# The second MLP of a three-layer kernel on one core: hidden units first and whole, then a down projection by seven block products

## The chip, the cores and the metric

One core of a Trainium2 chip. The metric is the device time of one execution in microseconds (us). TensorE is PE in the profile (its weight loads are PEld), VectorE is DVE, ScalarE is ACT, GpSimd is POOL, SyncE is SP.

## What is computed

Retention attention on q, k, v (2 batches, 8 heads, 768 positions, 64 per head) gives x of 2 x 768 x 512. Then a mixing layer and an MLP, cut to what matters:

```python
theta = x @ w_theta
y = einsum('ts,bsd->btd', w_tok_r, x * cos(theta)) + einsum('ts,bsd->btd', w_tok_i, x * sin(theta))
u = x + y
x = u + maximum(u @ w_ch, 0)                      # the channel layer
h = maximum(x.T @ w_tok1, 0) @ w_tok2             # per batch, over the 768 tokens, inner width 256
u = x + h.T
out = u + maximum(u @ w_ch1, 0) @ w_ch2           # the second MLP: 512 -> 1536 -> 512
```

## The kernel before

All activations stay on chip, channels on the partitions (NK = 4 blocks of 128), tokens along the free axis. Float32 operands are split in two parts, high (ACT, a rounding copy) and low (DVE or POOL, value less high), and each product is three matmuls of the parts: high by high, high by low, low by high (`three`, L780). Every engine's program is written out by hand in order, with semaphores between the engines.

In order of time: twelve attention chunks (g = 0 to 11) with theta, sine and cosine; the token mixing (`mix`), which is done with seven block products (STEPS = 28, 72 matmuls of 384 columns a product); the channel layer (`channels(q)`, q = 0 to 15), with turns of its result onto the other axis (`turn_x2`) from q = 9 on; `tokens_up`, `tokens_down`; and the second MLP.

In the attention start, ACT's first instruction of use is `x_high(0)` (L477), then two `theta_high` (L460); DVE does `x_low(0)` (L618) and two `theta_low` (L578), on which `theta(0)` of TensorE waits. `weigh(g)` (L594) multiplies the scores of a chunk by the decay.

`channels(0)` waits for y_kept of all 28 mixing steps, which DVE's `keep_y` (L687 at the end) signals.

The second MLP goes over three tiles of 512 tokens: batch 0's first 512, batch 1's first 512, and the last 256 of both. In each tile there are NF = 12 blocks of inner units. `hidden(tile, f)` makes one (12 matmuls of 512 columns into a PSUM bank), ACT takes its relu as high part (L561), DVE the low part (L768), and `down(tile, f)` adds its share to four banks of sums (12 matmuls of 512 columns), one block behind. After the 12th block DVE adds the four sums to res (L774) and SP sends them (L365).

Weights come in 17 pieces of 1024 columns through three stage buffers. ACT and DVE split the first five during the mixing, POOL splits the others (L373, L375): those of w_ch2 and w_ch1, in `w_a`, `ch2_a` and `w_b`. POOL also does the low parts `ut_low` (L400) ahead of the channel layer and `u2_low` (L406) ahead of the second MLP. In the mixing, POOL's queue makes sums of weight quarters by DMAs that add to what lies in `raw` (L420 to L437).

## Time and profile before

| | |
|---|---|
| median of 3 runs | 449.81 us (449.34 to 450.46) |
| profiled execution | 449.38 us, span 447.6 us |
| PE busy | 437.8 us, 98% of the span, 2676 matmuls |
| PEld busy | 382.3 us |
| DVE busy | 210.4 us |
| ACT busy | 127.9 us |
| POOL busy | 99.1 us |

The span is from the first to the last instruction of the profiled execution; its time holds 1.8 us more, which lies outside. Busy time of an engine is the union of its instructions. Consecutive matmuls overlap in the records (each lasts longer than the distance to the next), so the distance between starts is the price of one in a stream.

### The profile page before, as it was taken

To read this page: it belongs to the slowest core of one execution; us is meant where nothing else is said; L and a number is where in the kernel's file an instruction comes from. 1 tells how busy PE (TensorE), PEld (TensorE's weight loads), DVE (VectorE), ACT (ScalarE), POOL (GpSimd) and SP (SyncE) were. 2 spreads that over 40 slices of the span, in tenths; PEclk is the share of its full clock that TensorE was granted. 3 is DMA by queue.
4 is the path that set the end of the run, shared out by engine and by line. 5 is a ranking of instruction groups with operands and counts; after the bars stand their busy time and mean duration, and the time that the engine had idled before them with its cause. 6 is when DMAs were issued, how large, how long until landed. Compare 5 with 4: busy or idle time off the path is not lost.

```text
span 447.6 us, 6232 instructions
## 1 busy us (share of the span) xinstructions
PE 437.8 (98%) x2676; PEld 382.3 (85%) x2676; DVE 210.4 (47%) x304; ACT 127.9 (29%) x194; POOL 99.1 (22%) x80
## 2 busy tenths in 40 slices
PE   7799999999999999999999999999999999999996
PEld 4587878899999999999889888888888888888885
DVE  3789998799999993244335211112211113111113
ACT  0455654734455456012313211111111110111110
POOL 2422241000200009940998940000000000000000
PEclk9999999999999999999999999999999999999999
DMA  8955697540784111030241000000200001000002
GB/s 309 395 218 202 267 235 168 105 142 0 183 182 154 47 49 48 13 129 1 94 142 47 1 0 1 0 0 12 84 1 0 0 1 73 21 1 0 1 0 94
DMA packets 9980, 38.29 MB, mean 86 GB/s; under 512 B 993, under 2 KB 2145, under 8 KB 8161
## 3 DMA queue, kind: packets, MB, share of 16 engines
q1 hardware_dynamic: 7856, 28.31, 17.3%
q0 software_dynamic: 1952, 9.44, 9.2%
q8 instruction: 21, 0.34, 0.3%
q10 hardware_dynamic: 144, 0.14, 0.1%
q14 instruction: 7, 0.05, 0.0%
HBM read 34.75 MB, written 3.15 MB: 85 GB/s over the span
## 4 chain that ended last, share of the span: by engine, by line
PE 95%; DVE 2%; DMA 1%; ACT 1%; issue 0%; DVEq 0%; ACTq 0%
PE ps L780 85%; PE ps L797 3%; PE ps L837 3%; PE ps L851 2%; PE ps L927 1%; PE ps L811 1%; PE ps L827 1%; DMA qkv_in<-qkv 1%; DVE w_sq L578 1%; DVE res L774 1%; DVE prob L594 1%; ACT L477 0%; ACT w_sq L460 0%; ACT x_hi L477 0%; DVE res L613 0%
## 5 line engine op out<-in xcount | busy, mean ns | idle before, releaser
L780 PE MATMUL ps<-u,w_a 128*128 128x512 f32 x432 | 103.3, 389 | 0.0
L768 DVE SCALAR_TENSOR_TENSOR w_sq<-ps,w_sq 128x512 fp32r<-128x512 f32 x36 | 24.9, 692 | 156.7 <-ACT w_sq L561 156.7
L780 PEld LDWEIGHTS ps<-u,w_a 128*128 128x128 f32 x432 | 81.1, 188 | 16.8
L780 PE MATMUL ps<-tw,zs 128*128 128x384 f32 x504 | 88.1, 334 | 0.0
L780 PEld LDWEIGHTS ps<-tw,zs 128*128 128x128 f32 x504 | 87.3, 188 | 0.1
L561 ACT ACTIVATE w_sq<-ps 128x512 fp32r<-128x512 f32 x36 | 21.6, 599 | 168.0 <-PE ps L780 168.0
L780 PE MATMUL ps<-w_sq,ch_a 128*128 128x512 f32 x216 | 51.9, 389 | 0.0
L780 PE MATMUL ps<-w_sq,w_b 128*128 128x512 f32 x216 | 51.4, 389 | 0.0
L780 PEld LDWEIGHTS ps<-w_sq,w_b 128*128 128x128 f32 x216 | 40.5, 188 | 8.4
L780 PEld LDWEIGHTS ps<-w_sq,ch_a 128*128 128x128 f32 x216 | 40.5, 188 | 8.4
L780 PE MATMUL ps<-ut,w_sq 128*128 128x384 f32 x192 | 35.6, 339 | 0.7 <-issue 0.7
L504 ACT ACTIVATE zs<-z 128x768 fp32r<-128x768 f32 x28 | 23.7, 846 | 37.0 <-PE ps L780 37.0
L780 PEld LDWEIGHTS ps<-ut,w_sq 128*128 128x128 f32 x192 | 32.9, 188 | 1.0 <-issue 1.0
L780 PE MATMUL ps<-w_sq,x_hi 128*128 128x512 f32 x96 | 30.8, 402 | 2.3 <-DVE w_sq L578 2.3
L400 POOL TENSOR_TENSOR ut<-res,ut 128x384 fp32r<-128x384 f32 x16 | 16.6, 1068 | 33.0 <-ACT ut L509 33.0
L780 PEld LDWEIGHTS ps<-w_sq,x_hi 128*128 128x128 f32 x96 | 17.1, 188 | 5.9 <-issue 2.2
L584 DVE TENSOR_TENSOR tw<-raw,tw 128x768 fp32r<-128x768 f32 x21 | 20.8, 988 | 0.0
L780 PE MATMUL ps<-w_sq,x_lo 128*128 128x512 f32 x48 | 18.8, 392 | 0.0
L385 POOL TENSOR_TENSOR k_dec<-qkv_in,cst 128x512 f32<-128x512 f32 x10 | 11.5, 1148 | 30.7 <-DMA qkv_in<-qkv 26.8
L731 DVE SCALAR_TENSOR_TENSOR res<-ps,res 128x384 f32<-128x384 f32 x16 | 8.9, 558 | 19.3 <-PE ps L780 19.3
L467 ACT ACTIVATE tw<-raw 128x768 fp32r<-128x768 f32 x21 | 17.4, 830 | 1.0 <-DMA raw<-tok 1.0
L780 PE MATMUL ps<-u,w_b 128*128 128x512 f32 x72 | 17.4, 395 | 0.0
(83 smaller groups left out, 473.1 us busy)
## 6 DMA issues: line engine op xcount, KB each, us to landing
qkv_in<-qkv SPq DMA_DIRECT2D x11, 1024.0 KB, 6.1
stage<-weights SPq DMA_DIRECT2D x17, 512.0 KB, 3.3
raw<-tok POOLq DMA_DIRECT2D x7, 1152.0 KB, 8.9
cols_out<-res SPq DMA_DIRECT2D x12, 256.0 KB, 2.1
raw<-tok SPq DMA_DIRECT2D x6, 384.0 KB, 8.1
raw<-tok POOLq DMA_DIRECT2D x3, 384.0 KB, 9.2
qkv_in<-qkv SPq DMA_DIRECT2D x2, 512.0 KB, 5.0
raw<-theta_w SPq DMA_DIRECT2D x2, 512.0 KB, 8.6
```

The source lines that it names most:

```text
L385: pool.tensor_tensor(heads(k_dec[:, n % 2, :]), heads(qkv_in[:, g % NQ, 2 * DM:3 * DM]), key_decay, ALU.mult).then_inc(key_ready, 1)
L400: pool.tensor_tensor(u_half(1, b, k, half), res_half(b, k, half), f32(u_half(0, b, k, half)), ALU.subtract).then_inc(ut_lo, 1)
L467: act.activation(tw[:, p % 2, 0, at], raw[:, W_RAW[p], at], ACT.Copy).then_inc(tok_hi, 1)
L504: act.activation(zs[:, s % NZ, 0, :], z[:, Z_KIND[p], i, :], ACT.Copy, scale=Z_SIGN[p]).then_inc(z_hi, 1)
L561: act.activation(h2[:, f % 2, 0, :], bank(BK_H2 + f % 4), ACT.Relu).then_inc(h2_hi, 1)
L584: dve.tensor_tensor(tw[:, p % 2, 1, at], raw[:, W_RAW[p], at], f32(tw[:, p % 2, 0, at]), ALU.subtract).then_inc(tok_lo, 1)
L731: dve.scalar_tensor_tensor(out=part, in0=ps[:, BK_M + q % 2, 0:HS], scalar=0.0, in1=part, op0=ALU.max, op1=ALU.add).then_inc(x2_kept, 1)
L768: dve.scalar_tensor_tensor(out=h2[:, f % 2, 1, :], in0=bank(BK_H2 + f % 4), scalar=0.0, in1=f32(h2[:, f % 2, 0, :]), op0=ALU.max, op1=ALU. ...
L780: mm = pe.matmul(dst, left(l), right(r), start=first and n == 0, stop=last and n == 2, skip_group_check=True)
L797: mm = pe.matmul(ps[:, BK_SCORE + r, i * P:(i + 1) * P], qkv_in[rows, g % NQ, DM + i * P:DM + (i + 1) * P], qkv_in[rows, g % NQ, i * P:(i ...
L837: mm = pe.matmul(ps[cols, BK_Y + r, i // 2 * P:(i // 2 + 1) * P], qkv_in[:, g % NQ, 3 * DM + h * D:3 * DM + (h + 1) * D], prob[:, r, i * P ...
L851: mm = pe.transpose(ps[:, BK_XROW, k * P:(k + 1) * P], res[:, b, k, c * P:(c + 1) * P], ident)
```

## The change

Three edits.

1. ACT runs a sine over one column of the zeroed tile `idle` at its very start, before it waits for the constants.
2. The wait for y_kept of all 28 steps moves from `channels(0)` to `turn_x2(0)`.
3. The second MLP is in two parts. First all 36 `hidden` blocks (12 matmuls of 512 columns each, in the order of HIDDEN, eight PSUM banks in turn). ACT (`first_units`) keeps relu of batch 0, DVE (`second_units`) that of batch 1 less another block, unsplit, in `h_a` and `h_b`. Then seven products p, each of four cells i (an output block of 128 channels and 384 tokens), each cell of 6 x 3 = 18 matmuls of 384 columns. The inner axis is halved, the output channels are halved, and the batches are the third pair. Each product needs one operand of sums of hidden units (`h_sums`, DVE), split by `h_op_high` (ACT) and `h_op_low` (DVE) in six parts of 768 columns, and one operand of sums of w_ch2 quarters of 1536 columns, split by `w2_high` and `w2_low`. The sums of weights are made by POOL's adding DMAs in `w2_raw`. A cell's result is added by DVE (`keep_down`) to one or three places of res. Operands of product p + 1 are made while product p runs; each operand has two buffers. w_ch1 is no longer held whole: its six pieces go through the three places of `ch1`, the last three split by POOL when the places come free. There are 11 pieces; w_ch2 is loaded apart from them, 768 KB a quarter.

The constants are NPHI = NF // 2 = 6 and W2C = 2 * NPHI * P = 1536; MIDDLE, the first piece that POOL splits, is now P_CH1. `hidden_units(f_half, phi, b)` is a slice of `h_a` (phi below 4) or `h_b`; `h_op(p, phi)` one of 12 places in `h_ops_a`, `h_ops_b`, `h_ops_c`, the last of which lies over `u`. `parts_of(b, n)` counts the units of batch b kept by the first n blocks; `hidden_kept(eng, n)` waits for block n to have been taken from its bank.

```diff
+DOWN = 7
+CELLS = 4
+H_PLACE = ((0, 0), (1, 0), (1, 1), (0, 0), (1, 0), (0, 1), (0, 0))
+H_SUMS = (3, 4, 6)
+W2_RAW = (0, 1, 0, 1, 1, 1, 0)
+W2_SIGN = (1.0, 1.0, 1.0, -1.0, -1.0, 1.0, -1.0)
+HIDDEN = [(f, 0) for f in range(4)] + [(f, t) for f in range(4) for t in (1, 2)] + [
+    (f, t) for f in range(4, NF) for t in range(TILES)]
...
-BK_SUM, BK_H2 = 0, 4
+BK_H2 = (1, 2, 4, 5, 3, 6, 7, 0)
+BK_DOWN = (0, 0, 4, 4, 4, 0, 0)
...
             sp.wait_ge(zi_ready, NG)
             for i in range(N_PIECES):
                 load_piece(i)
-            for tile in range(TILES):
-                for n in range(NK):
-                    sp.wait_ge(sum_kept, tile * NK + n + 1)
-                    to = out[tile, n, :, 0:DM] if tile < B else out[:, n, :, DM:S].rearrange("b p t -> p b t")
-                    sp.dma_start(to, tokens(tile, n)).then_inc(out_sent, 16)
-            sp.wait_ge(out_sent, 16 * TILES * NK)
+            split_done(sp, N_PIECES - 1)
+            for i in range(2):
+                sp.dma_start(w2_raw[:, i, :], ch2[i]).then_inc(w2_in[i], 16)
+            for p, r, b in ((1, 0, 0), (4, 1, 0), (5, 1, 1), (6, 0, 1)):
+                for i in range(CELLS):
+                    m, half = i // 2, i % 2
+                    sp.wait_ge(down_kept, p * CELLS + i + 1)
+                    sp.dma_start(out[b, 2 * r + m, :, half * HS:(half + 1) * HS],
+                                 res_half(b, 2 * r + m, half)).then_inc(out_sent, 16)
+            sp.wait_ge(out_sent, 16 * 4 * CELLS)
...
                     for k in range(NK):
                         ut_low(b, k, half)
             pool.wait_ge(mix_ready, STEPS)
-            for i in range(P_CH2A, P_CH1):
...
+            for i in range(P_CH1, P_CH1 + NSTAGE):
                 split_piece(i)
             u2_low(0)
             u2_low(1)
...
+                f = 2 * (i - P_CH1 - NSTAGE) + 1
+                pool.wait_ge(h2_ready, HIDDEN.index((f, 2)) + 1)
                 split_piece(i)
+            def load_w2(i, q, sent):
+                pool.dma_start(w2_raw[:, i, :], ch2[q]).then_inc(sent, 16)
+            def add_w2(i, q, sent):
+                pool.dma_start(w2_raw[:, i, :], ch2[q], accum_op=ALU.add).then_inc(sent, 16)
+            pool.wait_ge(w2_lo, 1)
+            add_w2(0, 2, s2_part)
+            pool.wait_ge(s2_part, 16)
+            add_w2(0, 3, s2_w_in)
+            pool.wait_ge(w2_lo, 2)
+            load_w2(1, 0, w2_11_again)
+            pool.wait_ge(w2_11_again, 16)
+            add_w2(1, 2, s3_w_in)
+            pool.wait_ge(w2_lo, 3)
+            add_w2(0, 1, s4_w_in)
+            pool.wait_ge(w2_lo, 4)
+            load_w2(1, 3, w2_22_in)
+            pool.wait_ge(w2_lo, 5)
+            add_w2(1, 2, s1_w_in)
...
+            act.wait_ge(idle_ready, 1)
+            act.activation(spare[:, :], idle[:, 0:1], ACT.Sin)
             act.wait_ge(const_in, 16)
             for g in range(NG + 2):
...
-            def h2_high(tile, f):
-                act.wait_ge(h2_ready, tile * NF + f + 1)
-                act.activation(h2[:, f % 2, 0, :], bank(BK_H2 + f % 4), ACT.Relu).then_inc(h2_hi, 1)
+            def first_units(n):
+                f, tile = HIDDEN[n]
+                cols = slice(0, DM) if tile == 0 else slice(DM, S)
+                act.wait_ge(h2_ready, n + 1)
+                act.activation(hidden_units(f % 2, f // 2, 0)[:, cols], bank(BK_H2[n % 8])[:, 0:cols.stop - cols.start],
+                               ACT.Relu).then_inc(h2_first, 1)
+            def h_op_high(p, phi):
+                half, b = H_PLACE[p]
+                if p in H_SUMS:
+                    act.wait_ge(h_sum, H_SUMS.index(p) * NPHI + phi + 1)
+                elif b:
+                    act.wait_ge(h2_second, parts_of(1, HIDDEN.index((2 * phi + half, 2)) + 1))
+                else:
+                    act.wait_ge(h2_first, parts_of(0, HIDDEN.index((2 * phi + half, 2)) + 1))
+                if p == 1 or p == 0 and phi >= 4:
+                    act.wait_ge(h2_ready, len(HIDDEN))
+                elif p >= 2:
+                    act.wait_ge(down_ready, (p - 1) * CELLS)
+                act.activation(h_op(p, phi)[:, 0, :], hidden_units(half, phi, b), ACT.Copy).then_inc(h_op_hi, 1)
+            def w2_high(p):
+                act.wait_ge((w2_in[0], w2_in[1], s2_w_in, s3_w_in, w2_22_in, s1_w_in, s4_w_in)[p], 16)
+                if p == 0:
+                    act.wait_ge(h2_ready, HIDDEN.index((9, 2)) + 1)
+                elif p == 1:
+                    act.wait_ge(h2_ready, len(HIDDEN))
+                else:
+                    act.wait_ge(down_ready, (p - 1) * CELLS)
+                act.activation(w2[:, p % 2, 0, :], w2_raw[:, W2_RAW[p], :], ACT.Copy,
+                               scale=W2_SIGN[p]).then_inc(w2_hi, 1)
...
-            for tile in range(TILES):
-                for f in range(NF):
-                    h2_high(tile, f)
+            for n in range(len(HIDDEN)):
+                f, tile = HIDDEN[n]
+                if tile != 1:
+                    first_units(n)
+                if tile == 2 and f % 2 and f < 8:
+                    h_op_high(0, f // 2)
+                if (f, tile) == (10, 2):
+                    w2_high(0)
+            h_op_high(0, 4)
+            h_op_high(0, 5)
+            for p in range(1, DOWN):
+                w2_high(p)
+                for phi in range(NPHI):
+                    h_op_high(p, phi)
...
-                    dve.tensor_tensor(part, as_tokens(tile, bank(BK_SUM + n)), part, ALU.add).then_inc(sum_kept, 1)
+            def second_units(n):
+                f, tile = HIDDEN[n]
+                half, phi = f % 2, f // 2
+                cols, at = (slice(0, DM), 0) if tile == 1 else (slice(DM, S), S - DM)
+                less = hidden_units(0, phi, half)[:, cols]
+                dve.wait_ge(h2_ready, n + 1)
+                if tile == 2:
+                    dve.wait_ge(h2_first, parts_of(0, n + 1))
+                elif half == 0:
+                    dve.wait_ge(h2_first, parts_of(0, HIDDEN.index((f, 0)) + 1))
+                else:
+                    dve.wait_ge(h2_second, parts_of(1, HIDDEN.index((f - 1, 1)) + 1))
+                if tile == 2 and half:
+                    dve.wait_ge(h2_second, parts_of(1, HIDDEN.index((f - 1, 2)) + 1))
+                dve.scalar_tensor_tensor(out=hidden_units(half, phi, 1)[:, cols],
+                                         in0=bank(BK_H2[n % 8])[:, at:at + cols.stop - cols.start], scalar=0.0,
+                                         in1=less, op0=ALU.max, op1=ALU.subtract).then_inc(h2_second, 1)
+            def h_op_low(p, phi):
+                half, b = H_PLACE[p]
+                dve.wait_ge(h_op_hi, p * NPHI + phi + 1)
+                dve.tensor_tensor(h_op(p, phi)[:, 1, :], hidden_units(half, phi, b), f32(h_op(p, phi)[:, 0, :]),
+                                  ALU.subtract).then_inc(h_op_lo, 1)
+            def h_sums(p, phi):
+                t1, t2 = hidden_units(0, phi, 1), hidden_units(1, phi, 1)
+                to = hidden_units(*H_PLACE[p][:1], phi, 0)
+                dve.wait_ge(h_op_lo, (0, 0, 0, 0, 1, 0, 3)[p] * NPHI + phi + 1)
+                if p == 6:
+                    dve.tensor_tensor(to, t2, t1, ALU.add).then_inc(h_sum, 1)
+                else:
+                    dve.wait_ge(h2_second, parts_of(1, HIDDEN.index((2 * phi + 1, 2)) + 1))
+                    dve.tensor_tensor(to, t2, to, ALU.subtract).then_inc(h_sum, 1)
+            def w2_low(p):
+                dve.wait_ge(w2_hi, p + 1)
+                what, hi, lo = w2_raw[:, W2_RAW[p], :], w2[:, p % 2, 0, :], w2[:, p % 2, 1, :]
+                if W2_SIGN[p] > 0:
+                    dve.tensor_tensor(lo, what, f32(hi), ALU.subtract).then_inc(w2_lo, 1)
+                else:
+                    dve.scalar_tensor_tensor(out=lo, in0=what, scalar=-1.0, in1=f32(hi), op0=ALU.mult,
+                                             op1=ALU.subtract).then_inc(w2_lo, 1)
+            def keep_down(p, i):
+                m, half = i // 2, i % 2
+                r11, r12 = (res_half(b, m, half) for b in range(B))
+                r21, r22 = (res_half(b, 2 + m, half) for b in range(B))
+                got = ps[:, BK_DOWN[p] + i, 0:HS]
+                dve.wait_ge(down_ready, p * CELLS + i + 1)
+                if p == 0:
+                    dve.tensor_tensor(r12, r12, got, ALU.add)
+                    dve.tensor_tensor(r21, r21, got, ALU.subtract)
+                    dve.tensor_tensor(r22, r22, got, ALU.subtract).then_inc(down_kept, 1)
+                elif p == 1:
+                    dve.tensor_tensor(r11, r11, got, ALU.add).then_inc(down_kept, 1)
+                elif p == 2 or p == 6:
+                    dve.tensor_tensor(r12, r12, got, ALU.subtract).then_inc(down_kept, 1)
+                elif p == 4:
+                    dve.tensor_tensor(r21, r21, got, ALU.add).then_inc(down_kept, 1)
+                else:
+                    dve.tensor_tensor(r22, r22, got, ALU.add).then_inc(down_kept, 1)
+            for n in range(len(HIDDEN)):
+                f, tile = HIDDEN[n]
+                if tile != 0:
+                    second_units(n)
+                if tile == 2 and f % 2 and f < 8:
+                    h_op_low(0, f // 2)
+                    h_sums(3, f // 2)
+                if (f, tile) == (10, 2):
+                    w2_low(0)
+            h_op_low(0, 4)
+            h_op_low(0, 5)
...
+            later = {0: [(3, 4), (3, 5)], 1: [(4, 0), (4, 1), (4, 2)], 2: [(4, 3), (4, 4), (4, 5)],
+                     3: [(6, 0), (6, 1), (6, 2)], 4: [(6, 3), (6, 4), (6, 5)]}
+            for p in range(DOWN):
+                if p + 1 < DOWN:
+                    w2_low(p + 1)
+                if p:
+                    keep_down(p - 1, 3)
+                for phi in range(NPHI):
+                    if phi == 2:
+                        keep_down(p, 0)
+                    elif phi == 5:
+                        keep_down(p, 1)
+                    if p + 1 < DOWN:
+                        h_op_low(p + 1, phi)
+                for q, phi in later.get(p, ()):
+                    h_sums(q, phi)
+                keep_down(p, 2)
+            keep_down(DOWN - 1, 3)
...
                 half, b, n = q // (B * NK), q // NK % B, q % NK
                 if q == 0:
                     split_done(pe, P_T12 - 1)
-                    pe.wait_ge(y_kept, STEPS)
                 if q >= 2:
...
             def turn_x2(n):
                 b, c = turned(n)
                 pe.wait_ge(x2_kept, (n // 3 + 1) * NK)
+                if n == 0:
+                    pe.wait_ge(y_kept, STEPS)
...
-                if tile == 0 and f == 2:
...
+                if n == 4:
...
+                split_done(pe, P_CH1 + f // 2)
                 for k in range(NK):
-                    if tile < B and f == 0:
-                        pe.wait_ge(u2_lo, tile * NK + k + 1)
-                    at = (f * NK + k) * P
-                    mm = three(bank(BK_H2 + f % 4), lambda l: w_a[:, l, at:at + P],
+                    if f == 0:
+                        pe.wait_ge(u2_lo, (0 if tile == 0 else NK) + k + 1)
+                    at = (f % 2 * NK + k) * P
+                    mm = three(bank(BK_H2[n % 8]), lambda l: ch1[:, f // 2 % NSTAGE, l, at:at + P],
                                lambda r: u_tokens(tile, r, k), k == 0, k == NK - 1)
                 mm.then_inc(h2_ready, 1)
-            def down(tile, f):
-                pe.wait_ge(h2_lo, tile * NF + f + 1)
-                if tile == 0 and f >= NF // 2:
-                    split_done(pe, P_CH2B + (f - NF // 2) * DM // PIECE)
-                for n in range(NK):
-                    if tile and f == 0:
...
-                down(tile, NF - 1)
+            def down(p, i):
+                m, half = i // 2, i % 2
+                pe.wait_ge(w2_lo, p + 1)
+                if p in (1, 3, 4, 6):
+                    pe.wait_ge(down_kept, (p - 1) * CELLS + i + 1)
+                elif p == 5:
+                    pe.wait_ge(down_kept, CELLS + i + 1)
+                else:
+                    for n in range(len(HIDDEN) - 8, len(HIDDEN)):
+                        if BK_H2[n % 8] == BK_DOWN[p] + i:
+                            hidden_kept(pe, n)
+                for phi in range(NPHI):
+                    if i == 0:
+                        pe.wait_ge(h_op_lo, p * NPHI + phi + 1)
+                    at = (m * NPHI + phi) * P
+                    mm = three(ps[:, BK_DOWN[p] + i, 0:HS], lambda l: w2[:, p % 2, l, at:at + P],
+                               lambda r: h_op(p, phi)[:, r, half * HS:(half + 1) * HS],
+                               p in (0, 2, 5) and phi == 0, phi == NPHI - 1)
+                mm.then_inc(down_ready, 1)
+            for n in range(len(HIDDEN)):
+                hidden(n)
+            for p in range(DOWN):
+                for i in range(CELLS):
+                    down(p, i)
```

## Rows read from the trace of the kernel before

**Rows 1.** The page: busy us of each engine; a group of instructions (busy us, mean ns)

```profile
PE 437.8 (98%) x2676; PEld 382.3 (85%) x2676; DVE 210.4 (47%) x304; ACT 127.9 (29%) x194; POOL 99.1 (22%) x80
...
L375 POOL TENSOR_TENSOR w_a<-stage,w_a 128x1024 fp32r<-128x1024 f32 x6 | 14.4, 2400 | 0.5
```

**Rows 2.** The chain that ended last: start us, length us, what

```profile
11.63 1.28 ACT L477
...
91.18 84.25 PE ps L780 x486
...
176.13 12.73 PE ps L780 x72
...
219.19 222.80 PE ps L780 x1005
...
442.01 2.73 DVE res L774 x4
```

**Rows 3.** Timeline of TensorE in the second MLP: start us, length us, instructions

```profile
247.97 5.64 PE L780 MATMUL ps<-u,w_a 128*128 128x512 f32 x24
253.45 2.88 PE L780 MATMUL ps<-w_sq,ch_a 128*128 128x512 f32 x12
256.17 2.88 PE L780 MATMUL ps<-u,w_a 128*128 128x512 f32 x12
```

**Rows 4.** Timeline of all engines in the first 31 us

```profile
11.54 1.23 DVE L594 TENSOR_TENSOR prob<-ps,causal 128x1024 f32<-128x1024 f32 x1
...
13.59 0.69 DVE L618 TENSOR_TENSOR x_lo<-res,x_hi 128x512 fp32r<-128x512 f32 x1 [0.82 <-ACT x_hi L477]
...
14.86 1.80 POOL L385 TENSOR_TENSOR k_dec<-qkv_in,cst 128x512 f32<-128x512 f32 x1 [4.01 <-DMA qkv_in<-qkv]
...
26.36 1.28 ACT L494 ACT_TABLE_LOAD   x1
```

**Rows 5.** The tile raw: durations ns min/median/max of the theta low parts

```profile
L578 DVE SCALAR_TENSOR_TENSOR w_sq<-raw,w_sq x2: 1227/1647/2067, 14.5 to 15.7; 128x1024 fp32r<-128x1024 f32 x2
```

**Rows 6.** Timelines of PE, DVE and POOL around the channel layer's start

```profile
164.69 10.74 PE L780 MATMUL ps<-tw,zs 128*128 128x384 f32 x61
...
175.47 0.56 DVE L687 TENSOR_TENSOR res<-res,ps 128x384 f32<-128x384 f32 x1 [2.57 <-PE ps L780]
...
168.46 16.60 POOL L400 TENSOR_TENSOR ut<-res,ut 128x384 fp32r<-128x384 f32 x16 [33.02 <-ACT ut L509]
```

**Rows 7.** Busy time by window: us, PE, PEld, DVE, ACT, POOL, PEclk, DMA share, GB/s

```profile
91.20:175.40 84.20, 84.20 (x486) 83.91 (x485) 75.62 (x103) 44.20 (x61) 11.89 (x13) 1.00 0.37 107
...
116.20:128.70 12.50, 12.50 (x74) 12.50 (x73) 12.50 (x17) 6.66 (x8) 3.81 (x4) 1.00 0.87 163
```

**Rows 8.** Timeline of DVE in the mixing

```profile
125.11 1.22 DVE L590 TENSOR_TENSOR w_sq<-stage,w_sq 128x1024 fp32r<-128x1024 f32 x1
126.25 0.55 DVE L678 TENSOR_TENSOR res<-res,ps 128x384 f32<-128x384 f32 x1
126.71 0.95 DVE L649 TENSOR_TENSOR zs<-z,zs 128x768 fp32r<-128x768 f32 x1
127.58 0.95 DVE L661 TENSOR_TENSOR z<-z 128x768 f32<-128x768 f32 x1
```

**Rows 9.** Timeline of ACT in the mixing

```profile
123.24 1.04 ACT L471 ACTIVATE w_sq<-stage 128x1024 fp32r<-128x1024 f32 x1
...
128.73 0.85 ACT L504 ACTIVATE zs<-z 128x768 fp32r<-128x768 f32 x1 [0.44 <-PE ps L780]
129.48 0.83 ACT L467 ACTIVATE tw<-raw 128x768 fp32r<-128x768 f32 x1
```

**Rows 10.** DMA issues from POOL's queue at 110.8, 116.5 and 64.2 us: KB each, us to landing

```profile
raw<-tok POOLq DMA_DIRECT2D x1, 1152.0 KB, 5.5
...
raw<-tok POOLq DMA_DIRECT2D x1, 1152.0 KB, 9.0
...
raw<-tok POOLq DMA_DIRECT2D x1, 1152.0 KB, 12.2
```

More of the change, by code:

```diff
@@ L99, in retention_mixer_mlp @@
         cst = sb("cst", [P, N_CONST])
+        spare = sb("spare", [P, 1])
         res = sb("res", [P, B, NK, S])
-        w_sq = sb("w_sq", [P, 2, NK * DM], F32R)
+        with ExitStack() as middle:
+            w_sq = sb("w_sq", [P, 2, NK * DM], F32R, within=middle)
+        h_ops_a = sb("h_ops_a", [P, 3, 2, S], F32R)
         with ExitStack() as first:
@@ L172, in retention_mixer_mlp, with hidden_units, h_op @@
         h1 = w_sq[:, :, :].rearrange("p b (l j n) -> p b l j n", l=2, j=NT)
-        h2 = h1[:, 0]
-        def w_ch2(part, f, n):
-            w, f = (ch2_a, f) if f < NF // 2 else (w_b, f - NF // 2)
-            return w[:, part, f * DM + n * P:f * DM + (n + 1) * P]
+        def hidden_units(f_half, phi, b):
+            return h_a[:, phi, f_half, b, :] if phi < 4 else h_b[:, phi - 4, f_half, b, :]
+        def h_op(p, phi):
+            e = p % 2 * NPHI + phi
+            return (h_ops_a[:, e] if e < 3 else h_ops_b[:, 0] if e == 3 else h_ops_c[:, e - 4])
         def piece_home(i):
-            for start, w in ((P_CH2B, w_b), (P_CH1, w_a), (P_CH2A, ch2_a), (P_T12, w_b), (P_WCH, w_sq)):
+            if i >= P_CH1:
+                return [ch1[:, (i - P_CH1) % NSTAGE, part, :] for part in range(2)]
+            for start, w in ((P_T12, w_b), (P_WCH, w_sq)):
                 if i >= start:
@@ L278, in retention_mixer_mlp @@
         h2_ready = sem("h2_ready")
-        h2_hi = sem("h2_hi")
-        h2_lo = sem("h2_lo")
-        sum_ready = sem("sum_ready")
-        sum_kept = sem("sum_kept")
+        h2_first = sem("h2_first")
+        h2_second = sem("h2_second")
+        h_sum = sem("h_sum")
+        h_op_hi = sem("h_op_hi")
+        h_op_lo = sem("h_op_lo")
+        w2_in = [sem(f"w2_in{i}") for i in range(2)]
+        s2_part = sem("s2_part")
+        s2_w_in = sem("s2_w_in")
+        s4_w_in = sem("s4_w_in")
+        w2_11_again = sem("w2_11_again")
+        s3_w_in = sem("s3_w_in")
+        w2_22_in = sem("w2_22_in")
+        s1_w_in = sem("s1_w_in")
+        w2_hi = sem("w2_hi")
+        w2_lo = sem("w2_lo")
+        down_ready = sem("down_ready")
+        down_kept = sem("down_kept")
         def split_done(eng, i):
@@ L444, in _ @@
             pool.wait_ge(mix_ready, STEPS)
-            for i in range(P_CH2A, P_CH1):
-                split_piece(i)
-            pool.wait_ge(m_ready, 4 * NK)
-            for i in range(P_CH1, P_CH2B):
+            for i in range(P_CH1, P_CH1 + NSTAGE):
                 split_piece(i)
@@ L994, in _ @@
-            for tile in range(TILES):
-                for f in range(NF):
-                    hidden(tile, f)
-                    if f:
-                        down(tile, f - 1)
-                down(tile, NF - 1)
+            def down(p, i):
[17 more added lines that the diff above has]
+                mm.then_inc(down_ready, 1)
```

74 lines of the change are left out of this document (35 added, 39 removed).

## Prediction

> **What bounds the kernel now.** I read the page first: TensorE is busy for 98% of the span [rows 1]. The chain of waits says the same: but for the first 22 us, a gap before the channel layer and the last adds, it is TensorE's own matmuls one after another [rows 2]. So only three things can move the time: how many columns stream through TensorE, where TensorE stands still, and the tail. The second MLP is 432 + 432 = 864 matmuls of 512 columns. In the timeline twelve start 256.17 - 253.45 = 2.72 us apart, 0.2267 us each [rows 3]; from 247.97 this gives 195.8 us, up to 443.8.
>
> **Start.** ACT's first copy comes behind a load of its table, 11.63 to 12.91 [rows 2], and the first sine brings another load at 26.36 [rows 4]. After that one no third appears, although copies and relus follow: the sine's set holds them. With a sine in front there is one load, while ACT has nothing to do. The high part of x is then ready 1.28 us sooner, but DVE works on weigh(1) from 11.54 to 12.77, and its x_low had waited 0.82 us before 13.59 [rows 4]. So x_low starts at 12.77; the theta low parts behind it started at 14.5 after another 0.26 us of waiting for ACT, and win 1.1 us. The second low part took 2.07 us in place of 1.23 [rows 5] because POOL works beside it from 14.86 [rows 4]; POOL's start hangs on a DMA and stays where it is, so that part may come out no shorter, but its start moves. I take -1.1. Bounds: 0, if a chunk's landing sets TensorE's pace here, and -1.28. The second load lies beside TensorE's work: nothing.
>
> **Channel layer.** The mixing's last matmuls fill 61 x 0.1734 = 10.58 us from 164.69, so the next slot is 175.27; channels(0) starts at 176.13, just after the last keep_y (175.47 to 176.03) [rows 6]. Its other wait is for POOL's ut_low: the four of batch 0 are done at 168.46 + 4 x 1.04 = 172.6, so nothing is late behind the wait removed, -0.9. At turn_x2(0), nine channel blocks later, y_kept is long there: nothing. Bounds 0 and -0.9.
>
> **Down projection.** Removed: 432 matmuls at 0.2267 = 97.9 us. Added: 7 x 4 x 18 = 504 of 384 columns. The mixing has exactly these, with the same three-part order: 84.25 / 486 = 0.1734 us each [rows 2], so 87.4 us. That is -10.5. The saving in columns is one eighth (221,184 to 193,536), but both spacings are 13 ns above columns / 2.4 GHz, and more matmuls pay that more often. In the mixing, at a granted clock of 1.00, the weight loads are busy for 83.91 of 84.20 us [rows 7], so 384 columns stand near the point where the load would bind; the 0.1734 already has it. The Trainium skill (TensorE: Matmul & The Clock Gate, Back-to-back issue gap) gives N/2.4 + 2.5 ns for the isolated gap. By it the two would be 93.2 and 81.9 us, an estimate of -11.3; the traces show larger gaps, and I go by them.
>
> **Hidden blocks.** The 432 matmuls stay, at the same price. What TensorE waits for there: banks (eight now, so 8 x 2.72 us until one returns), and the ring of w_ch1. Its fourth piece may be split from block 8 on and is used at block 18: ten blocks, 27 us, for a split of 2.40 us [rows 1] and a copy of about 1.1. The next two are alike. u2_low of batch 1 is needed at block 4, 10.9 us after the first; POOL followed keep_u2 closely before and has less in front of it now. ACT and DVE have for each pair of inner blocks (16.3 us) under 3 and 4 us of work. Nothing, and if this cover went, 3.5 us per late piece.
>
> **The seam.** Operand parts phi 4 and 5 of product 0 can only be made when all hidden blocks are through, since they lie over u. Call T the end of the last hidden block's slots. From start to start of 768 columns DVE needs 0.87 us [rows 8], ACT 0.75 [rows 9]. ACT: last relu until T+0.6, high parts done at T+1.45 and T+2.2; DVE: last units, low parts done at T+2.45 and T+3.35. TensorE does phi 0 to 3 in 4 x 3 x 0.1734 = 2.1 us, waits 0.4, does phi 4, waits 0.4. I take +0.8; bounds 0 and +1.7 (every operation at its full length plus a wait of 0.1 each).
>
> **Does DVE keep up in the products?** This is the question of the change, as a product lasts 72 x 0.1734 = 12.5 us. DVE's spacings are 1.14 for 1024 columns, 0.87 for 768 and 0.46 for 384 [rows 8], a slope of 1.05 ns a column, so 1.68 for 1536. A product from p = 1 on: w2_low 1.68, six h_op_low 5.22, four keeps 1.8, three sums 2.6, in all 11.4 us. Product 0 has eight more adds and one sum less: 14.1. From w2_low(1) at about T+3.7 to the last operand of product 6 the queue holds 6 x 1.68 + 36 x 0.87 + 30 x 0.46 + 14 x 0.87 = 67.4 us, so it could be done by T+71.1; TensorE wants that last part at T + 6 x 12.48 + 0.8 + 2.6 = T+78.3. The tightest earlier places: the last part of product 2, there at T+25.8 and wanted at T+28.3; and the result of cell 2 of product 0, kept at T+16.5 and wanted at T+19.5, as product 1 adds on in that bank. In the mixing DVE had 12.5 us busy in 12.5 with no gap in TensorE [rows 7]. So nothing, with a slack of 10%. ACT has 1.4 + 6 x 0.75 = 5.9 us a product.
>
> **Weight sums.** A plain transfer of 1152 KB landed in 5.5 us, an adding one in 9.0, beside other loads in 12.2 [rows 10]; these are 768 KB, so I take 5 and 7, and 9.0 as the bound for a quiet queue. The first pair starts at T-4.3 and is in by T+11 to T+15; w2_high(2) wants it at T+13.3 and could take it at T+20. The pair for product 3 is in by about T+19 to T+25, wanted at T+25.7. The later ones have a product's length each. Nothing.
>
> **Tail.** Before: 443.8 to 447.6, 3.8 us. After: last cell's result 0.2 later, one add of 0.6 rather than 0.7, then the same 2.9 us for the send (447.6 less 442.01 + 2.73 [rows 2]). -0.2.
>
> **Sum.** -1.1 - 0.9 - 10.5 + 0.8 - 0.2 = -11.9. Against the profiled execution's own 449.38: 437.5. The median of the runs is 0.43 above that execution, so 437.9 for a median.
>
> **Rivals.**
> *DVE becomes the bound (slower).* Rows speak for it: with two operands in SBUF beside POOL's work, DVE took 2.07 us instead of 1.23, 1.69 times [rows 5]. If POOL's issuing of adding DMAs did that throughout, 67.4 us would become 114, 46 us more, less the slack of 7: about 477. It decides from 1.28 times: 67.4 x 0.28 = 19 = 7 slack + 11.9. Against it: between 116.2 and 128.7, with four POOL DMAs issued and the DMA share at 0.87, TensorE had no gap [rows 7], and 768 columns kept their 0.87 at 126.7. In the products POOL has no arithmetic at all. The Trainium skill (TensorEngine Tiling (Array Packing), PSUM Bottleneck) warns that after a saving on TensorE the copies out of PSUM may bind; here the mixing runs at that edge without a gap. A half case, 1.15 to 1.25 times: 441 to 448.
> *The weight sums come late.* With 12.2 us for each adding DMA and 9 for a plain one, s3 lands near T+32 instead of T+25.7 and the later links need d + 3.9 us each out of 12.5: 2 us lost at product 3 and some 5 after it, 444 to 445. Against it: no other load runs then.
> *The early sine gives nothing*, since landings bind the first chunks or a copy loads its set again: 439.0. For it: POOL waits for landings there [rows 4]; against: TensorE's own waits for chunks end well before.
>
> **How the numbers follow.** My forecast 0.70; sine worth nothing 0.11; sums late 0.06; DVE a little over its slack 0.08; DVE so slow that it decides 0.04; within 0.3% of before 0.01. 0.3% (1.35 us) is about what a measurement of this kernel can tell from no change. So faster 0.95, same 0.01, slower 0.04. The forecast's own range is 436.4 (full 1.28, no stall at the seam) to 438.9; the early half of the other cases takes the top to 441.5.
>
> **What would show it.** One ACT_TABLE_LOAD, in the first 3 us; theta's first matmuls some 1.1 us sooner; no gap at the channel layer; 504 matmuls with 0.173 us spacing; a stop of 0.8 us at the seam and no other; DVE close to 90% busy in the products but with waits for PE in it. I am wrong if TensorE waits for DVE's low parts from product 2 on, if w2_high waits for a DMA with TensorE behind it, if the granted clock falls after the seam, or if 384 columns take more than 0.175 us with these operands.

## The result and the profile after

| | before | after |
|---|---|---|
| median | 450.13 us (449.34 to 450.65, 4 runs) | 435.71 us (435.51 to 435.96, 4 runs) |
| profiled execution | 449.38 us, span 447.6 | 435.77 us, span 434.0 |

The ratio is 0.9681, 95% interval 0.9667 to 0.9694: 14.4 us less. The prediction was 437.9 us with a range of 436.4 to 438.9 for its own case. The measured median lies 0.7 us below that range: the direction was right and the forecast gain too small.

The page of the changed kernel answers to [rows 1]:

```profile
PE 426.8 (98%) x2748; PEld 388.3 (89%) x2748; DVE 278.4 (64%) x383; ACT 158.3 (36%) x231; POOL 85.3 (20%) x75
```

TensorE is still the bound. DVE has 68 us more work, and in the second MLP TensorE waits for it at one place only. The kernel's chain of waits answers to [rows 2]:

```profile
11.26 1.22 DVE prob L712
12.48 0.60 DVE x_lo L736
13.08 1.15 DVE w_sq L696
14.23 0.14 issue
14.36 3.01 PE ps L982 x12
...
216.13 126.91 PE ps L982 x582
...
343.35 0.84 ACT h_ops_c L657
344.19 0.02 issue
344.22 1.84 DVE h_ops_c L906 x2
346.06 0.04 issue
346.10 85.05 PE ps L982 x489
431.15 0.02 issue
431.17 0.56 DVE res L942
```

The table load is gone from the start; x_low follows the weighing without a wait, and all 12 matmuls of theta(0) run in one piece. There is no gap at the channel layer. At 343 us stands the seam: ACT's and DVE's work on operand parts 4 and 5. After it 489 matmuls run without a stop to the last add. The timeline of TensorE shows the seam as recorded:

```profile
244.91 20.38 PE L982 MATMUL ps<-u,ch 128*128 128x512 f32 x89
...
342.87 1.75 PE L982 MATMUL ps<-h_ops_a,w 128*128 128x384 f32 x9
344.45 0.69 PE L982 MATMUL ps<-h_ops_b,w 128*128 128x384 f32 x3
345.23 1.66 PE L982 MATMUL ps<-h_ops_c,w 128*128 128x384 f32 x6
346.73 1.72 PE L982 MATMUL ps<-h_ops_a,w 128*128 128x384 f32 x9
```

Three matmuls take 0.52 us, so part 4 was due at 344.97 and came at 345.23, 0.26 us late; six take 1.04, so the next cell was due at 346.27 and came at 346.73, 0.46 us late because of part 5. Together 0.72 us, where 0.8 was forecast.

The two spans differ by 13.6 us. Cut at three places that both traces have:

| stretch | before | after | measured | recorded |
|---|---|---|---|---|
| start, to the third group of scores | 19.38 | 17.30 | -2.08 | -1.1 |
| gap ahead of the channel layer | 0.86 | 0 | -0.86 | -0.9 |
| other work up to the second MLP | | | -0.12 | 0 |
| second MLP to its last matmul slot | 195.8 | 186.1 | -9.8 | -9.7 |
| from there to the span's end | 3.79 | 3.03 | -0.76 | -0.2 |

So the second MLP came out as worked out, and two small terms were too small: by 1.0 us at the start and by 0.56 at the tail. The median moved by 0.8 us more than these two executions; that is taken up below.

### The profile page after: what moved, and what is told of

Read it like the earlier page. It is cut to its first block, busy times and chain, and to the rows that moved or that the text cites. A ratio compares the mean times of both kernels' runs of the same rounds, so it can differ in the third digit from the quotient of the medians.

```text
span 434.0 us, 6621 instructions
## 1 busy us (share of the span) xinstructions
PE 426.8 (98%) x2748; PEld 388.3 (89%) x2748; DVE 278.4 (64%) x383; ACT 158.3 (36%) x231; POOL 85.3 (20%) x75
## 4 chain that ended last, share of the span: by engine, by line
PE 96%; DVE 2%; DMA 1%; ACT 0%; issue 0%; ACTq 0%; DVEq 0%
PE ps L982 85%; PE ps L999 3%; PE ps L1039 3%; PE ps L1053 2%; PE ps L1130 1%; PE ps L1013 1%; PE ps L1029 1%; DMA qkv_in<-qkv 1%; DVE prob L712 1%; DVE h_ops_c L906 0%; DVE w_sq L696 0%; ACT h_ops_c L657 0%; DVE x_lo L736 0%; DVE res L731 0%; DVE res L942 0%
## 5 line engine op out<-in xcount | busy, mean ns | idle before, releaser
L982 PE MATMUL ps<-u,ch 128*128 128x512 f32 x432 | 98.1, 389 | 0.0
L982 PEld LDWEIGHTS ps<-u,ch 128*128 128x128 f32 x432 | 81.1, 188 | 16.8
L982 PE MATMUL ps<-h_ops_c,w 128*128 128x384 f32 x312 | 57.0, 335 | 0.2
L982 PEld LDWEIGHTS ps<-h_ops_c,w 128*128 128x128 f32 x312 | 54.2, 188 | 0.8 <-DVE h_ops_c L906 0.8
L899 DVE SCALAR_TENSOR_TENSOR h_a<-ps,h_a 128x512 f32<-128x512 f32 (+1 forms) x16 | 8.9, 558 | 44.3 <-PE ps L982 26.3
L642 ACT ACTIVATE h_a<-ps 128x512 f32<-128x512 f32 (+1 forms) x16 | 7.9, 491 | 54.2 <-PE ps L982 54.2
L982 PE MATMUL ps<-h_ops_a,w 128*128 128x384 f32 x144 | 27.6, 334 | 0.0
L982 PEld LDWEIGHTS ps<-h_ops_a,w 128*128 128x128 f32 x144 | 25.2, 188 | 0.1
L460 POOL TENSOR_TENSOR u<-res,u 128x768 fp32r<-128x768 f32 x8 | 14.7, 1843 | 40.2 <-ACT u L636 40.2
L667 ACT ACTIVATE w<-w_raw 128x1536 fp32r<-128x1536 f32 x7 | 10.4, 1486 | 32.0 <-PE ps L982 32.0
```

Source lines behind the costliest of these rows:

```text
L460: pool.tensor_tensor(u[:, b, 1, k, :], res[:, b, k, :], f32(u[:, b, 0, k, :]), ALU.subtract).then_inc(u2_lo, 1)
L642: act.activation(hidden_units(f % 2, f // 2, 0)[:, cols], bank(BK_H2[n % 8])[:, 0:cols.stop - cols.start], ACT.Relu).then_inc(h2_first, 1)
L667: act.activation(w2[:, p % 2, 0, :], w2_raw[:, W2_RAW[p], :], ACT.Copy, scale=W2_SIGN[p]).then_inc(w2_hi, 1)
L899: dve.scalar_tensor_tensor(out=hidden_units(half, phi, 1)[:, cols], in0=bank(BK_H2[n % 8])[:, at:at + cols.stop - cols.start], scalar=0.0, ...
L982: mm = pe.matmul(dst, left(l), right(r), start=first and n == 0, stop=last and n == 2, skip_group_check=True)
```

## Experiments

Line numbers in the rows are each kernel's own. Times are compared with runs of the kernel before on the same chip; a variant of the changed kernel was not always on the chip of the changed kernel's own runs, so small differences between those two are read from the traces. The record has a mean granted clock for every execution, traced or not, and three levels of it come back below: 1.00 (0.999 or more), 0.996 (0.994 to 0.996) and 0.992 (0.991 or 0.992). `keep_warm(n, cols)` is n dummy matmuls of `cols` columns on the zeroed tile.

### The early sine alone

Added to the kernel before:

```diff
+            act.wait_ge(idle_ready, 1)
+            act.activation(spare[:, :], idle[:, 0:1], ACT.Sin)
             act.wait_ge(const_in, 16)
```

> The kernel before with the early sine alone. Theory A (the sine also takes DVE's second theta low part out of POOL's key product, which starts when a chunk lands): TensorE's third group of scores starts about 2 us sooner than at 19.38 us, the two theta low parts take about 2.4 us together and not 3.2, the time falls by 1.8 to 2.1 us. Theory B (the recorded step: only the wait for the table goes): 1.1 us less, the low parts still take 3.2 us. Theory C (the sine gives nothing, the missing time came from elsewhere): within 0.3 us of before.

Measured: 446.88 us against 449.59, ratio 0.9944 (0.9921 to 0.9967), 2.7 us less. DVE's timeline of this kernel, which answers to `14.53 3.21` in that of the kernel before (shown below):

```profile
12.22 0.68 DVE L621 TENSOR_TENSOR x_lo<-res,x_hi 128x512 fp32r<-128x512 f32 x1
12.82 2.35 DVE L581 SCALAR_TENSOR_TENSOR w_sq<-raw,w_sq 128x1024 fp32r<-128x1024 f32 x2
```

The two low parts take 2.35 us, not 3.21: both now run at 1.2 us. POOL's key product starts at 15.04, when they are nearly done (15.17). Theory A holds. Counted from the start of weigh(1), so that a different start of the execution doesn't enter, weigh(2) comes 7.23 us later and not 9.05: the sine is worth 1.8 us by this measure. Of it 0.86 is the collision avoided. B and C fall.

The median fell by 0.9 us more than these 1.8. The clocks of the executions say where to look: all 12 of this kernel have 1.00, and of the 29 of the kernel before 11 have. One of the 12 took 451.02 us at a clock of 1.00; no trace shows why.

What makes a collision slow is the order of the two instructions, which the rows of several traces show together. In each set below DVE's line is its two low parts, one behind the other. First the kernel before, where POOL starts within the first part; then the variant with two more DVE operations (below), where POOL starts within the second; then the later wait alone (below), where POOL starts 0.1 us ahead of the first:

```profile
14.53 3.21 DVE L578 SCALAR_TENSOR_TENSOR w_sq<-raw,w_sq 128x1024 fp32r<-128x1024 f32 x2 [0.26 <-ACT w_sq L460]
14.86 1.80 POOL L385 TENSOR_TENSOR k_dec<-qkv_in,cst 128x512 f32<-128x512 f32 x1 [4.01 <-DMA qkv_in<-qkv]
16.62 1.59 POOL L394 TENSOR_TENSOR carried<-state,cst 128x256 f32<-128x256 f32 x1
```

```profile
13.24 2.35 DVE L697 SCALAR_TENSOR_TENSOR w_sq<-raw,w_sq 128x1024 fp32r<-128x1024 f32 x2
14.70 1.79 POOL L440 TENSOR_TENSOR k_dec<-qkv_in,cst 128x512 f32<-128x512 f32 x1 [3.91 <-DMA qkv_in<-qkv]
```

```profile
14.92 1.04 POOL L385 TENSOR_TENSOR k_dec<-qkv_in,cst 128x512 f32<-128x512 f32 x1 [4.02 <-DMA qkv_in<-qkv]
15.03 3.56 DVE L578 SCALAR_TENSOR_TENSOR w_sq<-raw,w_sq 128x1024 fp32r<-128x1024 f32 x2 [0.26 <-ACT w_sq L460]
```

In the first set DVE's first part keeps its 1.23 us, POOL's product, which began within it, is drawn out from 1.04 to 1.80, and DVE's second part, which began within POOL's, takes 2.07. In the second set DVE and POOL overlap for 0.9 us, yet DVE keeps its 2.35 us and only POOL pays; in the third POOL keeps its 1.04 and DVE pays. In these traces the instruction that began first keeps its length, and the one that began second ends 0.90 us (POOL's product) or 1.08 us (a low part) after the end of the first.

### The later wait alone

```diff
 channels(q):   if q == 0:
                     split_done(pe, P_T12 - 1)
-                    pe.wait_ge(y_kept, STEPS)
 turn_x2(n): +  if n == 0:
             +      pe.wait_ge(y_kept, STEPS)
```

> The kernel before with the later wait alone. Recorded step: no gap between the mixing and the channel layer, 0.9 us less. Rival: another wait (a low part of the channel layer's operand) takes its place and the gap stays, 0 to 0.3 us less.

Measured: 449.02 us against 449.59, ratio 0.999 (0.9965 to 1.0016). The time cannot tell 0.9 us from nothing here. TensorE's timeline can:

```profile
164.74 12.99 PE L780 MATMUL ps<-tw,zs 128*128 128x384 f32 x74
177.57 4.67 PE L780 MATMUL ps<-ut,w_sq 128*128 128x384 f32 x26
```

The channel layer's first matmul starts at 177.57, which is 164.74 + 74 x 0.1734. No gap, and no other wait in its place.

### POOL's key product held back

```diff
 decay_keys(g):
                 pool.wait_ge(chunk_in[g % NQ], 16 * (g // NQ + 1))
+                if g == 2:
+                    pool.wait_ge(theta_lo, 2)
```

> The kernel before, with POOL's key product of chunk 2 held until both theta low parts are done; no sine, both table loads stay. Theory A: the second theta low part takes 1.2 us and not 2.07, the third group of scores starts 0.8 us sooner, about 0.8 us less in all; what POOL does later (carried state, wanted at 18.3 us) is just in time. Theory B or C (the collision of DVE and POOL has no part in it): no change, or slower by up to 1 us since POOL is late.

Measured: 448.87 us against 449.59, ratio 0.9981 (0.996 to 1.0002): the forecast size, but the interval reaches 1, so the time alone does not show it. The trace shows the step itself: low parts 2.36 us (13.66 to 16.02), POOL's product after them at 16.15. But the scores of chunk 2 came no sooner in this execution, for a reason that no theory had. TensorE's timeline:

```profile
15.03 0.85 PE L782 MATMUL ps<-w_sq,x_hi 128*128 128x512 f32 x2 [1.72 <-DVE w_sq L580]
15.68 0.63 PE L782 MATMUL ps<-w_sq,x_lo 128*128 128x512 f32 x1
16.11 1.06 PE L782 MATMUL ps<-w_sq,x_hi 128*128 128x512 f32 x2
```

After a stand of 1.7 us the same matmuls take 0.63 us in place of 0.39, and a pair 1.06 in place of 0.62. The windows of this kernel give the granted clock in the third last column:

```profile
10.00:12.00 2.00, 2.00 (x48) 1.67 (x46) 1.73 (x3) 1.25 (x1) 0.79 (x1) 1.00 1.07 434
12.00:22.00 10.00, 8.09 (x84) 6.11 (x76) 5.51 (x8) 3.79 (x6) 3.23 (x4) 0.83 1.00 403
```

0.83 over ten us is a third of them at the lower of the clock's two levels; from 16 to 18 us it is 0.50. This opened theory D, below.

### The new second MLP alone

The changed kernel less the two small edits (their diffs above, reversed).

> The changed kernel without the early sine and with the wait for all mixing steps back in front of the channel layer: the new second MLP alone. Theory A (the seven products give 9.7 us as recorded, and the last send standing alone gives 0.75 us, not 0.2): 10.4 to 10.6 us less than before. Rival (the products gave more than recorded because the start gave only 1.1): 11.4 us less or more. Start and gap as in the kernel before.

Measured: 439.92 us against 449.59, ratio 0.978 (0.9741 to 0.982), 9.7 us less, where 10.4 to 10.6 was expected; the interval, 8 to 11.6 us, holds both that and the rival's 11.4, so the time does not decide. The profiled execution too has a granted clock of 0.83 from 12 to 22 us. From the first hidden block to the span's end it takes 438.0 - 248.90 = 189.1 us; the changed kernel takes 434.0 - 244.91 = 189.1, the kernel before 447.6 - 247.97 = 199.6. The stage gives 10.5 us, tail included, in both kernels that have it, as theory A has it, whatever the start did. The rival falls by this. (One of the four executions took 440.74 us at a clock of 1.00; no trace shows why.)

### The last four sends together

```diff
-                    sp.wait_ge(down_kept, p * CELLS + i + 1)
+                    sp.wait_ge(down_kept, (p * CELLS + i if p < DOWN - 1 else DOWN * CELLS - 1) + 1)
```

> The changed kernel, with all four sends of product 6 issued only after its last cell is kept. Theory A (the tail is shorter because the last send no longer stands behind others: 2.3 us after the last add and not 2.9): the tail grows to 3.5 to 4.5 us, as four sends of 192 KB are issued some 0.4 us apart and share the DMA engines, so 1.2 to 2.2 us more in all. Rival (the tail is shorter only because a send is smaller, 192 KB and not 256): under 0.5 us more.

Measured: 437.32 us. By the trace, the last add ends at 430.81 + 0.55 = 431.4 and the span at 435.1: 3.7 us, where the changed kernel has 434.0 - 431.73 = 2.3. From the first hidden block to the end it is 435.1 - 244.52 = 190.6 us, 1.5 more. That is the time of theory A, but not for its reason. The last send is issued at 432.7, 1.3 us after the last add, because the other three are issued ahead of it; it then lands in 2.0 us, where the changed kernel's last one, issued 0.1 us after the last add and 3.1 us behind the one before it, lands in 1.8. Company costs 0.2 us here, and the order of issue 1.2. In the kernel before the last four sends, of 256 KB, leave 0.7 us apart and the last lands in 2.4 us; the fastest of 256 KB in that kernel took 2.0. So of the 0.6 us between 2.4 and 1.8 the rival, the smaller send, has a part (2.0 against 1.8 for the fastest of each size), and how the rest is shared is not shown.

### One and two more DVE operations in each product

```diff
                     if p + 1 < DOWN:
                         h_op_low(p + 1, phi)
+                        if phi < 1:        # second kernel: phi < 2
+                            more_work(p, phi)
+            def more_work(p, phi):
+                n = p * 1 + phi            # second kernel: p * 2 + phi
+                if n:
+                    dve.wait_ge(more_done, n)
+                dve.tensor_tensor(cst[:, 0:S], hidden_units(1, phi, 1), hidden_units(1, phi, 1),
+                                  ALU.subtract).then_inc(more_done, 1)
```

> The changed kernel with one more DVE operation of 768 columns (two inputs in SBUF, into constants no longer used) in each of products 0 to 5. By the recorded slack (7 us over the whole, 2.5 us at the last operand part of product 2) 6 x 0.87 = 5.2 us is hidden: no change, within 0.3 us. Rival (DVE is already at the bound, the slack is smaller than worked out): 2 to 5 us more.

> The changed kernel with two more such DVE operations in each of products 0 to 5, 10.4 us in all. By the recorded slack: DVE's part of a product becomes 13.1 us against TensorE's 12.5; TensorE waits 0.9 us at product 2 and 0.6 us at each of products 3 to 6, 3.3 us more in all (2.5 to 4.5). Rival (the slack is larger, as DVE overlaps more than the distances of the mixing show): under 1 us more. Rival (already at the bound): 8 to 10 us more.

With one: 436.74 us in the median of four, two at a clock of 1.00 (435.68 and 436.15) and two at 0.996 (437.33 and 437.73); the profiled execution has 435.68 and a span of 433.9. Its chain of waits again has one piece of matmuls from the seam to the end, 0.02 us longer than the changed kernel's:

```profile
345.99 85.07 PE ps L992 x489
431.06 0.02 issue
431.08 0.55 DVE res L950
```

So 5.2 us of DVE work cost nothing, with DVE busy without a break in five windows of a product's length, one behind the other. With two: 439.38 us, span 437.5, of which the second MLP has 437.5 - 245.16 = 192.3 us, 3.3 more than the changed kernel; 3.3 was worked out from the spacings. TensorE's waits for DVE stand where they were expected, one in each of products 2 to 6, and the chain of waits goes through DVE from the seam to product 6. Both rivals fall: DVE's slack is about 7 us over the stage (10.4 added less 3.3 lost), as recorded. Two windows of this kernel of a product's length, PE first and DVE third:

```profile
384.20:396.60 12.40, 12.09 (x70) 11.77 (x69) 12.40 (x16) 4.52 (x7) 0.85 (x1) 1.00 0.35 64
396.60:409.10 12.50, 12.20 (x71) 11.88 (x70) 12.50 (x16) 6.36 (x8) 0.00 (x0) 1.00 0.05 18
```

### Product 0 in two sweeps

```diff
-            for p in range(DOWN):
+            for phis in (range(4), range(4, NPHI)):
+                for i in range(CELLS):
+                    down(0, i, phis)
+            for p in range(1, DOWN):
                 for i in range(CELLS):
                     down(p, i)
 DVE, product 0: keep_down(0, 0) ahead of h_op_low(1, 5), keep_down(0, 1) behind it
```

> The changed kernel with product 0 done in two sweeps over its cells, operand parts 0 to 3 first and 4 and 5 after, so that TensorE has 8.3 us of work while parts 4 and 5 are made; DVE takes up the cells' results somewhat later. Recorded step (the stop at the seam is the wait for these two parts, 0.7 us): both stops go, 0.7 us less. Rival (the results of product 0, now ready only from 9.4 us on, make DVE late for product 1 or 2): the same 0.7 us or more appears at product 1 or 2, no gain or slower.

Measured: 434.95 us, span 432.9. The chain of waits has one piece from the token stage to the last add:

```profile
215.77 214.30 PE ps L984 x1086
430.07 0.02 issue
430.09 0.55 DVE res L942
```

From the first hidden block to the end: 432.9 - 244.54 = 188.4, 0.7 less than the changed kernel. The stop was the wait for parts 4 and 5, as recorded.

### Dummy matmuls in the stand ahead of theta(0)

```diff
                 if g == 1:
+                    keep_warm(2, DM)
                     theta(0)
```

in the kernel before.

> The kernel before with two dummy float32 matmuls of 512 columns on the zeroed tile put ahead of theta(0), where TensorE stands for some 2 us; nothing else. Theory D (in a part of the executions of every kernel without the early sine, that stand is followed by matmuls at half the clock for some 4 us, which makes the times scatter from 448.0 to 452.1 us; the sine shortens the stand to 0.7 us and so also ends this): no stretch below a granted clock of 1.00 at 16 to 22 us, the times lie within about 1 us, the median 0.5 to 1.5 us below that of before. Rival (the scatter has another cause, as the clock's rise before the first scores): median and scatter as before.

Measured: 448.7 us against 450.32, ratio 0.9964 (0.9947 to 0.9982). The granted clock is 1.00 in all windows of the start. But so it is in the profiled execution of the kernel before, so these two traces do not show what the clock is worth. From weigh(1) to weigh(2) it is 8.17 us here and 9.05 there, because this time DVE's second low part (at about 14.9) began before POOL's product:

```profile
13.74 2.36 DVE L578 SCALAR_TENSOR_TENSOR w_sq<-raw,w_sq 128x1024 fp32r<-128x1024 f32 x2 [0.25 <-ACT w_sq L460]
15.13 1.87 POOL L385 TENSOR_TENSOR k_dec<-qkv_in,cst 128x512 f32<-128x512 f32 x1 [4.02 <-DMA qkv_in<-qkv]
```

The mean clocks of all executions do speak for the clock: 9 of 12 have 1.00, against 3 of 17 of the kernel before on this chip. So half of theory D holds: matmuls that compute nothing take 1.6 us off the median, and the fall of the clock becomes rarer. The other half does not: three executions still have 0.996 (449.6 to 450.3 us), and those at 1.00 fall in two groups, six at 448.1 to 448.4 and three at 449.0 to 449.2. The groups lie as far apart as the order of DVE and POOL is worth, 0.9 us, and the kernel before at 1.00 has the same two, 448.0 to 448.7 and 449.2 to 449.4. That this order makes them is likely and not shown: of each kernel one execution was traced.

### The changed kernel again

> The changed kernel itself, as a control for the variants sent with it and before: 435.5 to 436.0 us, with few executions over 1 us above the fastest.

Measured: 437.35 us (435.8 to 437.54, 6 runs) against 450.32, ratio 0.9704 (0.9679 to 0.9729). One execution at 435.8, with a clock of 1.00; five at 437.3 to 437.5, outside the expectation, with 0.996, a group that the four runs of the result, all at 1.00, never showed. The profiled one (span 435.7) belongs to the slower group. Its windows:

```profile
7.50:10.00 2.50, 1.68 (x16) 1.68 (x18) 0.77 (x1) 0.00 (x0) 0.54 (x1) 0.62 0.99 415
10.00:12.00 2.00, 2.00 (x32) 1.88 (x30) 0.73 (x2) 0.00 (x0) 1.03 (x1) 0.63 1.07 440
```

The clock fell behind the first scores, after TensorE's stand of 1.5 us for the first weighing; after a stand of 1.4 us there the result's profiled execution kept 1.00. So weigh(1) starts at 12.47 and not 11.26, POOL's product begins before the second theta low part again, and the second MLP starts at 246.68 in place of 244.91:

```profile
14.22 3.20 DVE L696 SCALAR_TENSOR_TENSOR w_sq<-raw,w_sq 128x1024 fp32r<-128x1024 f32 x2
15.00 1.34 POOL L439 TENSOR_TENSOR k_dec<-qkv_in,cst 128x512 f32<-128x512 f32 x1 [3.91 <-DMA qkv_in<-qkv]
```

From there on it is the changed kernel, 435.7 - 246.68 = 189.0 us.

### A reordered start

The two sweeps, and: POOL's `carry_state(1)` ahead of `decay_keys(2)`, that one held for theta_lo as above, and

```diff
                 if g == 1:
-                    theta(0)
+                    theta(0, range(0, 2))
                 if g + 1 < NG:
                     scores(g + 1)
+                if g == 1:
+                    theta(0, range(2, NK))
```

> The changed kernel with product 0 in two sweeps (as tried alone: 0.7 us), and at the start: POOL's carried state of chunk 1 ahead of its key product of chunk 2, that product held until the theta low parts are done, and the scores of chunk 2 between the two halves of theta(0), so that the third weighing does not wait for them. The weighing of chunk 2 starts some 1.5 us sooner than at 18.5 us, after which TensorE's own work binds: 0.3 to 0.6 us more than the seam's 0.7, 1.0 to 1.3 us less than the changed kernel. Rival (the landing of chunk 2 at about 15 us or TensorE's work binds there already): no more than the seam's 0.7 us.

Measured: 434.87 us, against 434.95 for the sweeps alone. The weighing of chunk 2 did start at 16.81, but TensorE has work from 14.04 to 20.5 us without a stop, and outputs(2), its matmuls on the weighed chunk 2, starts 8.56 us after weigh(1), where the changed kernel has 19.79 - 11.26 = 8.53. The rival was right: DVE's answer was no longer what TensorE waited for.

### Both stands filled

The two sweeps, `keep_warm(1, DM)` behind scores(0) and `keep_warm(1, DM // 2)` ahead of theta(0).

> The changed kernel with product 0 in two sweeps, and TensorE's two stands at the start filled with dummy matmuls on the zeroed tile: one of 512 columns behind the first scores (a stand of 1.4 us), one of 256 ahead of theta(0) (0.7 us). Theory D, widened (each stand can be followed by a stretch at a lower clock, which in the control made 437.4 us of 435.8 in five of six executions): granted clock 1.00 throughout, all executions within 0.6 us of each other, 434.7 to 435.3 us. Rival (the fall at 7.5 to 12 us comes from what TensorE did before the first scores, not from the stand behind them): two groups of times 1.6 us apart remain.

Measured: 434.85 us (434.75 to 435.29, 5 runs) against 449.82, ratio 0.9673 (0.9652 to 0.9693). Granted clock 1.00 from 7.5 to 22 us, and 1.00 in the mean of all five executions, which lie within 0.54 us. That fits the theory; but the sweeps alone had 1.00 in three of four executions (434.69 to 435.08, and 436.02 with 0.996), so five executions do not prove that the slower group is gone.

## Why the prediction was wrong

**Start, the step that failed.** "POOL's start hangs on a DMA and stays where it is, so that part may come out no shorter, but its start moves. I take -1.1." The first half was right (POOL at 15.00 for 14.86), the conclusion not. The low parts start at 13.00 and are over at 15.35; POOL's product at 15.00 begins after the second low part has begun and does not lengthen it. The rows for that were there. The first low part, from 14.53, took 1.23 us although POOL began at 14.86, within it; the second, which began at 15.7, behind POOL, took 2.07 [rows 4, rows 5]. Moved by 1.1 us the second begins at about 14.6, ahead of 14.86, and so keeps 1.2 us: 1.1 + 0.84 = 1.9 by the recorded rows. I carried the slow duration along with the moved start. Measured, the term is 1.8 us by the sine. The other 0.3 us of the table above is luck: weigh(1) itself began 0.28 us sooner in this execution (11.26 for 11.54), as the first scores ran 1.6 us and not 2.1, for a reason that no run shows. My lower bound of -1.28, the length of the table load, was no bound: an instruction that moves can also shorten another by leaving its company.

**Tail.** I let "the same 2.9 us for the send" stand. It was 2.3. The last send of the kernel before is larger and has three others just issued beside it; the new one is smaller and alone. The together-sent variant shows 0.2 us for the company; how the 0.6 us are shared between company and size stays open.

**The median.** I added 0.43 us, the distance of the profiled execution from the median before. That distance comes from the start's scatter. In all series of runs the kernel before lies between 448.0 and 452.1 us, and the time goes with the mean granted clock: 448.0 to 449.4 at 1.00, 449.4 to 450.7 at 0.996, 451.8 to 452.1 at 0.992. The profiled execution before is of the first level, and its median, 449.81, lies where only the second has times; the four executions of the result are all at 1.00. In the control the median of the changed kernel was 437.35, inside my range: that the result fell below it is in part luck, of which executions were drawn. The gain is 3.0 to 3.2% in either series all the same.

**The account.** 437.9 less 435.7 is 2.2 us: 1.0 at the start, 0.56 at the tail, 0.4 of the median, and 0.2 of small differences. The bottom of the range was also added up wrongly. From 437.9, a start of 1.28 and no stall give 436.9; 436.4 comes out only without the 0.43 of the median.

**What held.** Gap: 0.86 us, no wait in its place. Products: 0.1734 us a matmul, 9.8 us with the seam. Seam: 0.72 for 0.8. Hidden blocks: 432 matmuls from 244.91 to 342.87, 0.2268 us each. DVE: no stall; 68.4 us busy over six windows of a product's length, where I had worked out 67.4 for the queue, and one and two more operations cost 0 and 3.3 us. Weight sums: the five adding DMAs landed in 6.7 to 7.0 us, where I took 7. The three rivals fell. The two added operations, which make 1.15 times DVE's work, cost 3.3 us.

## What to carry to other kernels

When a step moves, look up anew what runs beside it and which of the two begins first: its duration in the trace belongs to its old company, and the gain can be larger than the wait removed. Work out an engine's slack in a stage from the distances between starts, and test it by adding one and then two operations; here that gave the stall to a tenth of a microsecond. Before a median is forecast from one profiled execution, ask what makes the executions differ, and compare executions with the same granted clock.

## What the runs showed of the hardware

TensorE's granted clock falls, in some executions of the same kernel and not in others, behind stands of 1.5 to 2.6 us at the start: 0.62 from 7.5 to 12 us in one execution of the changed kernel, 0.83 from 12 to 22 us in those of three kernels without the early sine (the later wait, POOL held back, the new second MLP alone), 1.00 in those of two others. Matmuls then take 0.63 us for 0.39. With dummy matmuls in the stand the clock stayed at 1.00 in the profiled executions of both kernels that had them, and in 9 of 12 executions in place of 3 of 17 in the kernel before. Why one execution falls and the next does not stays open.

Where DVE's theta low parts and POOL's key product, each with two inputs in SBUF, overlap in these traces, the one that began first keeps its length and the other is drawn out: from 1.22 up to 2.07 us for DVE's 1024 columns, from 1.04 up to 1.87 for POOL's 512.

The best version tried, with product 0 in two sweeps and both stands filled, ran 434.85 us; the sweeps alone, 434.95, cannot be told from it.
